# Who makes the low parts while the weights are split: a token mixer and two feed-forward networks in split fp32 on one core

## The chip, the cores and the metric

The kernel runs on one core of a Trainium2 chip. The metric is the device time of one execution in microseconds; a median of several executions is given. The profile is that of one further execution.

## What is computed

```python
w   = softmax over the 7 taps of weight            # 8 heads x 7 taps
x   = causal 7-tap mix of x along the sequence     # (2, 4096, 192), a head has 24 channels
g   = x @ w_gate;  v = x @ w_val                   # 8192 x 192 @ 192 x 1536
x   = (g * sigmoid(g) * v) @ w_out                 # 1536 x 192: the first network
h   = x @ w_in                                     # 192 x 2048
out = where(h > 0, h, exp(min(h, 0)) - 1) @ w_out2 # 2048 x 192: the second network
```

All in fp32. TensorE multiplies fp32r operands, so each fp32 operand is split into a high part, which is the value converted to fp32r, and a low part, the value less the high part. A product is then made of three: high x high, low x high and high x low.

## The kernel before

**Tiling.** The 8192 tokens go in 16 chunks of 512. For a chunk the seven taps are applied on VectorE (`mix`), the result is split into the input of the first network, which has 12 blocks of 128 hidden rows, and the output of that is split into the input of the second network, with 16 blocks worked in 8 pairs. The code calls the first network of chunk n `mix_phase(n)`, because the taps of chunk n + 1 are applied beside it, and its second `elu_phase(n + 1)`. The order is mix_phase(0), mix_phase(1), elu_phase(1) (the second network of chunk 0), mix_phase(2), and a loop over the rest. The stretch from about 90 to 129 us of the trace is elu_phase(1), chunk 0's second network.

**One block of the first network.** TensorE projects gate and value into two PSUM banks (`project`, 18 matmuls of 512 columns); ScalarE makes the silu of the gate (line 557); VectorE multiplies it with the value into `hidden` (line 734, 128x512, two buffers); ScalarE converts that into `hid_hi` (line 574, a ring of four); an engine subtracts the two into `hid_lo` (a ring of four; GpSimd, line 441); TensorE multiplies both with the output weights three blocks later (`down1`, 10 matmuls). The bank of block f is free for block f + 2 once its product is made.

**One pair of the second network.** TensorE projects two blocks. VectorE takes the minimum with 0 of both (line 771), ScalarE the exponential (line 593), VectorE the ELU of both (line 787), ScalarE the high parts (line 608), GpSimd the low parts (line 441). `down2_pair` multiplies a pair two pairs later (32 matmuls). A pair's projection waits for the ELUs of the pair two before.

**The weights** come in 18 pieces of at most 768 columns through six staging buffers. Of each piece ScalarE makes the high part (`make_hi`, line 319) and GpSimd the low part (`make_lo`, line 326); one piece, out2's third (index 16), is VectorE's. Five pieces are made ahead of block 0, and the others "beside" certain blocks: a table names the block after whose own work both engines do which piece.

```python
BESIDE0 = {1: 5, 3: 6, 5: 7, 7: 8, 8: 9}              # first network of chunk 0
BESIDE1 = {0: 10, 1: 11, 9: 12, 10: 13, 11: 14}       # first network of chunk 1
BESIDE_ELU1 = {3: 15, 4: 16, 5: 17}                   # pairs of the second network
```

TensorE waits for the first n pieces, high and low, ahead of the block that first reads them (`wait_weights`): in elu_phase(1) piece 15 ahead of pair 6's projection, piece 16 ahead of the down pair of blocks 8 and 9, piece 17 ahead of that of 12 and 13 in mix_phase(2).

**The order** on each engine is that of its code; engines wait for each other by counting semaphores. In chunk 0 VectorE does, per block, the product and two tap instructions of chunk 1 (blocks 2 to 8), and the halo copy at block 9. ScalarE makes the high halves of chunk 1's input after block 9's high part, when all of `mix` is done (`input1_hi`, line 515), VectorE then its low halves (`input1_lo`, line 696), and SyncE copies the first half of each crosswise (`cross1`, line 365). In elu_phase(1) ScalarE makes the same high halves for chunk 2 after the high parts of blocks 8 and 10, VectorE the low halves after the minimums of pairs 5 and 6. GpSimd sums halves of the first network's output between its low parts (`sum_y_tail`, `sum_y_main`, `fold_y_tail`, line 445). SyncE's queue issues in order the loads of weights and of x; the load of chunk 2's x waits until the transposes of chunk 1's (`transpose_x`, line 708) have read the buffer.

Of the kernel before, what the change touches and what calls it, by code (L numbers as in the profile page):

```python
# [22 lines left out]
F32 = mybir.dt.float32  # L23
# [8 lines left out]
def mix_ffn_ffn(nc, x, weight, w_gate, w_val, w_out1, w_in2, w_out2, out):  # L32
# [39 lines left out]
    with ctx:  # L72
# [119 lines left out]
        piece_lo_dve = sem("piece_lo_dve")  # L192
        piece_lo_pool = sem("piece_lo_pool")
# [51 lines left out]
        def up1_piece(g, who):  # L245
# [4 lines left out]
            pieces.append((loads, [(hi, s)], [(lo, s, hi)], who))  # L250

        def up2_piece(j0, j1, who):
# [4 lines left out]
            pieces.append((loads, [(hi, s)], [(lo, s, hi)], who))  # L257

        def out_piece(rows, dst, q, order, who):
# [4 lines left out]
            pieces.append((loads, [(t[:, :, 0:D], s)], los, who))  # L264

        def out1_piece(q):
            out_piece(wo1_rows, out1_w, q, [(D, P, TAIL), (D + TAIL, 0, P)], "pool")

        UP1_AT, OUT1_AT = {}, {}
        for what, at, who in (("up", 0, "pool"), ("up", 1, "pool"), ("up", 2, "pool"), ("out", 0, "pool"),  # L270
                              ("up", 3, "pool"), ("up", 4, "pool"), ("out", 1, "pool"), ("up", 5, "pool"),
                              ("up", 6, "pool"), ("out", 2, "pool")):
            if what == "up":
                up1_piece(at, who)
# [7 lines left out]
        for what, at, who in (("up", 0, "pool"), ("up", 2, "pool"), ("out", 0, "pool"), ("up", 4, "pool"),  # L282
                              ("out", 1, "pool"), ("up", 6, "pool"), ("out", 2, "dve"), ("out", 3, "pool")):
            if what == "up":
                up2_piece(at, at + 2, who)
                UP2_AT[at] = len(pieces)
            else:
                out_piece(wo2_rows, out2_w, at, [(D, 0, D)], who)
                OUT2_AT[at * OT] = len(pieces)

        AHEAD, READY = 6, 5
        BESIDE0 = {1: 5, 3: 6, 5: 7, 7: 8, 8: 9}
        BESIDE1 = {0: 10, 1: 11, 9: 12, 10: 13, 11: 14}
        BESIDE_ELU1 = {3: 15, 4: 16, 5: 17}
        assert READY + len(BESIDE0) == PIECES1
# [5 lines left out]
        def lo_count(upto, who):  # L301

            return sum(len(p[2]) for p in pieces[:upto] if p[3] == who)

        def wait_weights(eng, upto):

            eng.wait_ge(piece_hi, upto)
            for who, made in (("dve", piece_lo_dve), ("pool", piece_lo_pool)):
                if lo_count(upto, who):
                    eng.wait_ge(made, lo_count(upto, who))  # L310
# [10 lines left out]
        def make_lo(eng, i, who):  # L321
            if pieces[i][3] != who:
                return
            eng.wait_ge(piece_hi, i + 1)
            for dst, src, hi in pieces[i][2]:
                ins = eng.tensor_tensor(dst, src, hi.bitcast(F32), ALU.subtract)  # L326
                ins.then_inc(piece_lo_dve if who == "dve" else piece_lo_pool, 1)
# [91 lines left out]
        def _(pool):  # L419
# [44 lines left out]
            def mix_phase(n, extra=lambda f: None):  # L464
                for f in range(N1):
                    pool.wait_ge(hi1_done, N1 * n + f + 1)
                    lo_of(f % 2, f % RING).then_inc(lo1_done, 1)
                    if f == 2 and is_int(n, 1):
                        sum_y_tail(0)
                    if f == 3 and is_int(n, 1):  # L470
                        sum_y_main(0)
                    if f == 6 and is_int(n, 1):
                        fold_y_tail(0)
                    extra(f)

            def elu_phase(n, extra=lambda j: None):
                last = is_int(n, CHUNKS)
                for k in range(N2 - last):
                    pool.wait_ge(hi2_done, N2 * (n - 1) + k + 1)
                    lo_of(k % 2, k % RING).then_inc(lo2_done, 1)  # L480
                    if k == 3 and not last:
                        sum_y_tail(n)
                    if k == 5 and not last:
                        sum_y_main(n)
                    if k == 9 and not last:
                        fold_y_tail(n)
                    if k % 2:
                        extra(k // 2)

            for i in range(READY):  # L490
                make_lo(pool, i, "pool")
            lo = lambda i: make_lo(pool, i, "pool")
# [167 lines left out]
        def _(v):  # L660
# [60 lines left out]

            def mix_phase(n):
                lead = isinstance(n, int)
                for f in range(N1):
# [119 lines left out]
            elu_phase(1, beside(BESIDE_ELU1, lambda i: make_lo(v, i, "dve")))  # L844
# [258 lines left out]
```

## Time and profile before

| | us |
|---|---|
| median of 3 runs (lowest, highest) | 1205.79 (1205.67, 1207.7) |
| the profiled execution | 1206.76 |
| its span in the trace | 1205.0 |
| TensorE matmuls busy | 1199.5 (100%) |
| VectorE busy | 775.5 (64%) |
| ScalarE busy | 664.2 (55%) |
| GpSimd busy | 717.9 (60%) |

The span is the time from the first to the last instruction of the trace; the execution's own time has 1.76 us around it. The granted clock of TensorE is 1.0 of full speed throughout. Busy shares are averages over stages; a wait of TensorE shows as idle time in front of a row of its timeline, with the instruction that released it.

### The profile page before, as it was taken

The numbers are of one execution on the slowest core, as the hardware profiler recorded it, in microseconds if no ns is written. First come the engines' busy times: TensorE is split into PE (matmuls) and PEld (weight loads), VectorE is DVE, ScalarE is ACT, GpSimd is POOL, SyncE is SP. The second block draws the span as 40 slices with busy tenths as digits, with TensorE's granted clock in tenths as the row PEclk, the third lists the DMA queues.
The fourth block names the chain that finished last, engine by engine and source line by source line (L and its number), as shares of the span: only waits on it lengthen the run. The fifth ranks groups of instructions, "written<-read, shape, count | busy, mean of one in ns | idle before, by whom it ended". The sixth has DMA issues, their size and how long they took to land.

```text
span 1205.0 us, 31390 instructions
## 1 busy us (share of the span) xinstructions
PE 1199.5 (100%) x11798; PEld 1032.4 (86%) x11798; DVE 775.5 (64%) x1178; ACT 664.2 (55%) x1114; POOL 717.9 (60%) x528
## 2 busy tenths in 40 slices
PE   9999999999999999999999999999999999999999
PEld 7988888888888888889888898888988889888898
DVE  6787575675656756567665666656666476675665
ACT  6456555465554645546455464655546556465565
POOL 6787656574654746547465474654746557465565
PEclk9999999999999999999999999999999999999999
DMA  7412012120111211012110121100212002120110
GB/s 179 109 51 44 12 27 41 32 44 11 32 31 30 44 30 23 21 30 44 30 27 17 30 44 30 35 17 22 44 30 41 11 22 44 30 44 9 30 34 15
DMA packets 103955, 43.37 MB, mean 36 GB/s; under 512 B 75888, under 2 KB 93936, under 8 KB 103920
## 3 DMA queue, kind: packets, MB, share of 16 engines
q1 hardware_dynamic: 103104, 42.29, 15.7%
q10 hardware_dynamic: 816, 0.59, 0.2%
q8 instruction: 24, 0.39, 0.1%
q14 instruction: 11, 0.09, 0.0%
HBM read 16.12 MB, written 6.29 MB: 19 GB/s over the span
## 4 chain that ended last, share of the span: by engine, by line
PE 97%; POOL 1%; DVE 1%; issue 1%; ACT 0%; ACTq 0%; DVEq 0%
PE up L860 55%; PE down L860 42%; POOL hid_lo L441 1%; DVE mixed L830 0%; DVE act L771 0%; PE down L1063 0%; POOL up_w_lo L326 0%; DVE hidden L787 0%; ACT L617 0%; ACT hid_hi L608 0%; POOL y_main L445 0%; POOL halves L445 0%; DVE mixed L827 0%; DVE taps_head L813 0%; ACT act L593 0%
## 5 line engine op out<-in xcount | busy, mean ns | idle before, releaser
L441 POOL TENSOR_TENSOR hid_lo<-hidden,hid_hi 128x512 fp32r<-128x512 f32 x447 | 623.7, 1405 | 473.2 <-ACT hid_hi L574 304.8
L860 PE MATMUL down<-out_w,hid_hi 64*128 64x384 f32 x2040 | 300.4, 355 | 0.0
L734 DVE TENSOR_TENSOR hidden<-act,up 128x512 f32<-128x512 f32 x191 | 130.8, 685 | 249.1 <-ACT act L557 249.1
L860 PE MATMUL down<-out_w,hid_lo 64*128 64x192 f32 x2040 | 260.8, 251 | 0.3 <-POOL hid_lo L441 0.3
L771 DVE TENSOR_SCALAR act<-up 128x512 f32<-128x512 f32 x256 | 164.8, 685 | 112.0 <-PE up L860 112.0
L860 PE MATMUL up<-in_b_hi,up_w_hi 64*128 64x512 f32 x1128 | 224.1, 393 | 0.0
L860 PE MATMUL up<-in_b_hi,up_w_lo 64*128 64x512 f32 x1128 | 223.7, 393 | 0.0
L860 PE MATMUL up<-in_b_lo,up_w_hi 64*128 64x512 f32 x1128 | 223.6, 393 | 0.0
L574 ACT ACTIVATE hid_hi<-hidden 128x512 fp32r<-128x512 f32 x192 | 121.5, 633 | 177.9 <-DVE hidden L734 160.5
L608 ACT ACTIVATE hid_hi<-hidden 128x512 fp32r<-128x512 f32 x256 | 156.9, 628 | 96.5 <-DVE hidden L787 79.4
L593 ACT ACTIVATE act<-act 128x512 f32<-128x512 f32 x256 | 156.1, 631 | 94.8 <-DVE act L771 94.8
L860 PEld LDWEIGHTS down<-out_w,hid_lo 64*128 64x128 f32 x2040 | 196.1, 187 | 6.1 <-POOL hid_lo L441 0.6
L557 ACT ACTIVATE act<-up 128x512 f32<-128x512 f32 x191 | 114.0, 597 | 155.5 <-PE up L860 153.6
L860 PEld LDWEIGHTS down<-out_w,hid_hi 64*128 64x128 f32 x2040 | 192.6, 184 | 5.4 <-issue 0.3
L787 DVE SCALAR_TENSOR_TENSOR hidden<-act,up 128x512 f32<-128x512 f32 x256 | 168.8, 680 | 34.4 <-POOL hid_lo L441 25.4
L860 PE MATMUL down<-hid_hi,out_w 64*128 64x512 f32 x1152 | 165.4, 391 | 0.0
L860 PE MATMUL up<-in_a_hi,up_w_hi 64*128 64x512 f32 x786 | 159.7, 398 | 0.4 <-DVE hidden L787 0.4
L860 PE MATMUL up<-in_a_lo,up_w_hi 64*128 64x512 f32 x786 | 156.8, 391 | 0.0
L860 PE MATMUL up<-in_a_hi,up_w_lo 64*128 64x512 f32 x786 | 156.2, 389 | 0.0
L690 DVE SCALAR_TENSOR_TENSOR mixed<-x_t,taps,mixed 128x512 f32<-128x512 f32 x192 | 146.2, 802 | 0.0
L860 PEld LDWEIGHTS down<-hid_hi,out_w 64*128 64x128 f32 x1152 | 110.5, 186 | 24.7 <-issue 0.4
L860 PEld LDWEIGHTS up<-in_b_lo,up_w_hi 64*128 64x128 f32 x1128 | 106.8, 185 | 24.6
(96 smaller groups left out, 1085.9 us busy)
## 6 DMA issues: line engine op xcount, KB each, us to landing
x_raw<-x_dram SPq DMA_DIRECT2D x136, 64.0 KB, 2.2
out_dram<-stage SPq DMA_DIRECT2D x15, 384.0 KB, 2.7
in_b_hi<-in_b_hi SPq DMA_DIRECT2D x32, 128.0 KB, 2.3
in_b_lo<-in_b_lo SPq DMA_DIRECT2D x32, 128.0 KB, 2.3
swapped<-halves SPq DMA_DIRECT2D x32, 128.0 KB, 2.3
in_a_hi<-in_a_hi SPq DMA_DIRECT2D x30, 128.0 KB, 2.3
in_a_lo<-in_a_lo SPq DMA_DIRECT2D x30, 128.0 KB, 2.3
stage<-w_out_dram SPq DMA_DIRECT2D x7, 384.0 KB, 3.9
```

Source lines behind the costliest of these rows:

```text
L441: return pool.tensor_tensor(hid_lo[:, slot, :], hidden[:, s, :], hid_hi[:, slot, :].bitcast(F32), ALU.subtract)
L557: nc.scalar.activation(act[:, f % 2, :], gate_bank(f, n)[:, :], ACT.Silu)\
L574: nc.scalar.activation(hid_hi[:, f % RING, :], hidden[:, f % 2, :], ACT.Copy)\
L593: nc.scalar.activation(act[:, k % 2, :], act[:, k % 2, :], ACT.Exp).then_inc(exp_done, 1)
L608: nc.scalar.activation(hid_hi[:, k % RING, :], hidden[:, k % 2, :], ACT.Copy)\
L690: v.scalar_tensor_tensor(mixed[:, part, :], src, tap, mixed[:, part, :], ALU.mult, ALU.add).then_inc(mix_step, 1)
L734: v.tensor_tensor(hidden[:, f % 2, :], act[:, f % 2, :], val_bank(f, n)[:, :], ALU.mult)\
L771: v.tensor_scalar(act[:, k % 2, :], elu_bank(k)[:, :], 0.0, None, ALU.min)\
L787: v.scalar_tensor_tensor(hidden[:, k % 2, :], act[:, k % 2, :], -1.0, elu_bank(k)[:, :], ALU.add, ALU.max).then_inc(elu_done, 1)
L860: return nc.tensor.matmul(dst, lhsT, rhs, start=start, stop=stop, skip_group_check=True)
```

## The change

In chunk 0's first network the low parts of all 12 blocks are made by VectorE (`chunk0_lo`), each after the next block's product, the last after block 11; GpSimd leaves them out. The transposes of chunk 1's x go from block 1 to block 2, the two taps per block from blocks 2 to 8 to blocks 3 to 9; the halo copy stays at block 9. Piece 5 is made beside block 2 instead of block 1.

In elu_phase(1) the low parts of pairs 3, 4 and 5 (blocks 6 to 11) are made by VectorE, one pair later: after the minimums (and the input's low half) of pairs 4, 5 and 6 and before their ELUs. GpSimd leaves them out. Piece 16 goes from VectorE to GpSimd, and all low parts of weights are counted by one semaphore, `piece_lo`, instead of two.

```diff
-        BESIDE0 = {1: 5, 3: 6, 5: 7, 7: 8, 8: 9}
+        BESIDE0 = {2: 5, 3: 6, 5: 7, 7: 8, 8: 9}
...
+        DVE_LO1 = (3, 4, 5)
...
         def wait_weights(eng, upto):
             eng.wait_ge(piece_hi, upto)
-            for who, made in (("dve", piece_lo_dve), ("pool", piece_lo_pool)):
-                if lo_count(upto, who):
-                    eng.wait_ge(made, lo_count(upto, who))
+            eng.wait_ge(piece_lo, lo_count(upto))
...
 # GpSimd, mix_phase
-                    pool.wait_ge(hi1_done, N1 * n + f + 1)
-                    lo_of(f % 2, f % RING).then_inc(lo1_done, 1)
+                    if not is_int(n, 0):
+                        pool.wait_ge(hi1_done, N1 * n + f + 1)
+                        lo_of(f % 2, f % RING).then_inc(lo1_done, 1)
...
 # GpSimd, elu_phase
-                    pool.wait_ge(hi2_done, N2 * (n - 1) + k + 1)
-                    lo_of(k % 2, k % RING).then_inc(lo2_done, 1)
+                    if not (is_int(n, 1) and k // 2 in DVE_LO1):
+                        pool.wait_ge(hi2_done, N2 * (n - 1) + k + 1)
+                        lo_of(k % 2, k % RING).then_inc(lo2_done, 1)
...
 # VectorE, mix_phase
+            def chunk0_lo(f):
+                v.wait_ge(hi1_done, f + 1)
+                lo_of(f).then_inc(lo1_done, 1)
...
                     v.tensor_tensor(hidden[:, f % 2, :], act[:, f % 2, :], val_bank(f, n)[:, :], ALU.mult)\
                         .then_inc(mul_done, 1)
+                    if is_int(n, 0) and f >= 1:
+                        chunk0_lo(f - 1)
...
-                    if f == 1 and is_int(n, 0):
+                    if f == 2 and is_int(n, 0):
                         transpose_x(1, 0)
                         transpose_x(1, 1)
...
-                    at = 2 if is_int(n, 0) else 3
-                    if f == at - 1:
+                    if f == 2:
                         mix(n + 1, 0)
-                    if at <= f < at + TAPS:
-                        mix(n + 1, 2 * (f - at) + 1)
-                        mix(n + 1, 2 * (f - at) + 2)
-                    if f == at + TAPS:
+                    if 3 <= f < 3 + TAPS:
+                        mix(n + 1, 2 * (f - 3) + 1)
+                        mix(n + 1, 2 * (f - 3) + 2)
+                    if f == (9 if is_int(n, 0) else 10):
                         mix(n + 1, MIX - 1)
...
+                if is_int(n, 0):
+                    chunk0_lo(N1 - 1)
...
 # VectorE, elu_phase, after the minimums and input1_lo, before the ELUs
+                    for k in (2 * j - 2, 2 * j - 1):
+                        if is_int(n, 1) and k // 2 in DVE_LO1:
+                            v.wait_ge(hi2_done, k + 1)
+                            lo_of(k).then_inc(lo2_done, 1)
...
-            elu_phase(1, beside(BESIDE_ELU1, lambda i: make_lo(v, i, "dve")))
+            elu_phase(1)
```

## Rows read from the trace of the kernel before

**Rows 1.** The page, engines: busy us (share of the span) xinstructions.

```profile
PE 1199.5 (100%) x11798; PEld 1032.4 (86%) x11798; DVE 775.5 (64%) x1178; ACT 664.2 (55%) x1114; POOL 717.9 (60%) x528
```

**Rows 2.** Timeline of TensorE, chunk 0: start us, us, engine line operation [idle before <-releaser].

```profile
22.17 0.40 PE L860 MATMUL up<-in_a_lo,up_w_hi 64*128 64x512 f32 x2
22.59 0.96 PE L860 MATMUL down<-hid_hi,out_w 64*128 64x512 f32 x6
...
23.82 0.42 PE L860 MATMUL up<-in_a_hi,up_w_hi 64*128 64x512 f32 x2
...
27.07 0.44 PE L860 MATMUL up<-in_a_hi,up_w_hi 64*128 64x512 f32 x2
...
49.88 0.91 PE L860 MATMUL down<-hid_hi,out_w 64*128 64x512 f32 x6
...
51.05 0.45 PE L860 MATMUL up<-in_b_hi,up_w_hi 64*128 64x512 f32 x2
```

**Rows 3.** Timeline of TensorE, chunk 0's second network.

```profile
109.78 0.44 PE L860 MATMUL up<-in_a_hi,up_w_hi 64*128 64x512 f32 x2
...
114.17 0.44 PE L860 MATMUL up<-in_a_hi,up_w_hi 64*128 64x512 f32 x2
...
116.28 0.39 PE L860 MATMUL down<-out_w,hid_hi 64*128 64x384 f32 x2
...
119.19 0.50 PE L860 MATMUL up<-in_a_hi,up_w_hi 64*128 64x512 f32 x2 [0.40 <-DVE hidden L787]
...
122.32 0.36 PE L860 MATMUL down<-out_w,hid_lo 64*128 64x192 f32 x2 [0.31 <-POOL hid_lo L441]
...
124.23 0.42 PE L860 MATMUL up<-in_b_hi,up_w_hi 64*128 64x512 f32 x2
```

**Rows 4.** Timeline of VectorE, chunk 0's second network.

```profile
107.70 1.29 DVE L771 TENSOR_SCALAR act<-up 128x512 f32<-128x512 f32 x2 [0.94 <-PE up L860]
...
112.50 3.63 DVE L326 TENSOR_TENSOR out_w<-stage,out_w 128x768 fp32r<-128x768 f32 x1 [1.97 <-ACT out_w L319]
...
117.26 0.68 DVE L696 TENSOR_TENSOR in_b_lo<-mixed,in_b_hi 128x512 fp32r<-128x512 f32 x1
```

**Rows 5.** Timeline of VectorE, chunk 0.

```profile
39.77 1.40 DVE L690 SCALAR_TENSOR_TENSOR mixed<-x_t,taps,mixed 128x512 f32<-128x512 f32 x2
...
46.18 1.77 DVE L696 TENSOR_TENSOR in_b_lo<-mixed,in_b_hi 128x512 fp32r<-128x512 f32 x1 [0.70 <-ACT in_b_hi L515]
```

**Rows 6.** Timeline of GpSimd, chunk 0.

```profile
46.11 1.30 POOL L326 TENSOR_TENSOR out_w<-stage,out_w 128x512 fp32r<-128x512 f32 x1
47.37 1.74 POOL L441 TENSOR_TENSOR hid_lo<-hidden,hid_hi 128x512 fp32r<-128x512 f32 x1
```

**Rows 7.** Timeline of GpSimd, chunk 0's second network.

```profile
111.51 2.56 POOL L441 TENSOR_TENSOR hid_lo<-hidden,hid_hi 128x512 fp32r<-128x512 f32 x2
114.01 1.30 POOL L445 TENSOR_TENSOR y_tail<-halves,swapped 128x512 f32<-128x512 f32 x1
...
122.23 1.85 POOL L326 TENSOR_TENSOR out_w<-stage,out_w 128x768 fp32r<-128x768 f32 x1
```

**Rows 8.** Timeline of SyncE's queue of DMA issues, chunk 0.

```profile
20.96 5.16 SPq L345 DMA_DIRECT2D x_raw<-x_dram  x8
...
47.98 1.11 SPq L365 DMA_DIRECT2D in_b_lo<-in_b_lo  x2
```

**Rows 9.** The page, DMA issues: engine op xcount, KB each, us to landing.

```profile
in_b_lo<-in_b_lo SPq DMA_DIRECT2D x32, 128.0 KB, 2.3
```

**Rows 10.** Timeline of ScalarE, chunk 0.

```profile
21.03 0.58 ACT L557 ACTIVATE act<-down 128x512 f32<-128x512 f32 x1
```

**Rows 11.** Timeline of ScalarE, chunk 0's second network.

```profile
107.33 0.83 ACT L319 ACTIVATE up_w_hi<-stage 128x768 fp32r<-128x768 f32 x1
...
110.60 0.61 ACT L515 ACTIVATE in_b_hi<-mixed 128x512 fp32r<-128x512 f32 x1
...
111.64 0.83 ACT L319 ACTIVATE out_w<-stage 128x768 fp32r<-128x768 f32 x1
```

More of the change, by code:

```diff
@@ L191, in mix_ffn_ffn @@
         piece_hi = sem("piece_hi")
-        piece_lo_dve = sem("piece_lo_dve")
-        piece_lo_pool = sem("piece_lo_pool")
+        piece_lo = sem("piece_lo")
         gate_ready = sem("gate_ready")
@@ L243, in mix_ffn_ffn, with up1_piece @@
         pieces = []
-        def up1_piece(g, who):
+        def up1_piece(g):
             c0, c1 = GROUPS[g]
@@ L249, in up1_piece, with up2_piece @@
             hi, lo = up1_w["hi"][:, :, c0:c1], up1_w["lo"][:, :, c0:c1]
-            pieces.append((loads, [(hi, s)], [(lo, s, hi)], who))
-        def up2_piece(j0, j1, who):
+            pieces.append((loads, [(hi, s)], [(lo, s, hi)]))
+        def up2_piece(j0, j1):
             s = stage[:, len(pieces) % STAGES, 0:PARTS * (j1 - j0) * P].rearrange("p (g c) -> p g c", g=PARTS)
@@ L256, in up2_piece, with out_piece @@
             hi, lo = up2_w["hi"][:, :, j0 * P:j1 * P], up2_w["lo"][:, :, j0 * P:j1 * P]
-            pieces.append((loads, [(hi, s)], [(lo, s, hi)], who))
-        def out_piece(rows, dst, q, order, who):
+            pieces.append((loads, [(hi, s)], [(lo, s, hi)]))
+        def out_piece(rows, dst, q, order):
             s = stage[:, len(pieces) % STAGES, 0:OT * D].rearrange("p (f d) -> p f d", d=D)
@@ L263, in out_piece @@
             los = [(t[:, :, to:to + n], s[:, :, of:of + n], t[:, :, of:of + n]) for to, of, n in order]
-            pieces.append((loads, [(t[:, :, 0:D], s)], los, who))
+            pieces.append((loads, [(t[:, :, 0:D], s)], los))
         def out1_piece(q):
-            out_piece(wo1_rows, out1_w, q, [(D, P, TAIL), (D + TAIL, 0, P)], "pool")
+            out_piece(wo1_rows, out1_w, q, [(D, P, TAIL), (D + TAIL, 0, P)])
         UP1_AT, OUT1_AT = {}, {}
-        for what, at, who in (("up", 0, "pool"), ("up", 1, "pool"), ("up", 2, "pool"), ("out", 0, "pool"),
-                              ("up", 3, "pool"), ("up", 4, "pool"), ("out", 1, "pool"), ("up", 5, "pool"),
-                              ("up", 6, "pool"), ("out", 2, "pool")):
+        for what, at in (("up", 0), ("up", 1), ("up", 2), ("out", 0),
+                         ("up", 3), ("up", 4), ("out", 1), ("up", 5), ("up", 6), ("out", 2)):
             if what == "up":
-                up1_piece(at, who)
+                up1_piece(at)
                 UP1_AT[GROUPS[at][0] // P] = len(pieces)
@@ L281, in mix_ffn_ffn @@
         UP2_AT, OUT2_AT = {}, {}
-        for what, at, who in (("up", 0, "pool"), ("up", 2, "pool"), ("out", 0, "pool"), ("up", 4, "pool"),
-                              ("out", 1, "pool"), ("up", 6, "pool"), ("out", 2, "dve"), ("out", 3, "pool")):
+        for what, at in (("up", 0), ("up", 2), ("out", 0), ("up", 4),
+                         ("out", 1), ("up", 6), ("out", 2), ("out", 3)):
             if what == "up":
-                up2_piece(at, at + 2, who)
+                up2_piece(at, at + 2)
                 UP2_AT[at] = len(pieces)
             else:
-                out_piece(wo2_rows, out2_w, at, [(D, 0, D)], who)
+                out_piece(wo2_rows, out2_w, at, [(D, 0, D)])
                 OUT2_AT[at * OT] = len(pieces)
         AHEAD, READY = 6, 5
-        BESIDE0 = {1: 5, 3: 6, 5: 7, 7: 8, 8: 9}
+        BESIDE0 = {2: 5, 3: 6, 5: 7, 7: 8, 8: 9}
         BESIDE1 = {0: 10, 1: 11, 9: 12, 10: 13, 11: 14}
         BESIDE_ELU1 = {3: 15, 4: 16, 5: 17}
+        DVE_LO1 = (3, 4, 5)
         assert READY + len(BESIDE0) == PIECES1
@@ L299, in beside, with lo_count @@
             return lambda at: make(table[at]) if at in table else None
-        def lo_count(upto, who):
-            return sum(len(p[2]) for p in pieces[:upto] if p[3] == who)
+        def lo_count(upto):
+            return sum(len(p[2]) for p in pieces[:upto])
         def wait_weights(eng, upto):
             eng.wait_ge(piece_hi, upto)
-            for who, made in (("dve", piece_lo_dve), ("pool", piece_lo_pool)):
-                if lo_count(upto, who):
-                    eng.wait_ge(made, lo_count(upto, who))
+            eng.wait_ge(piece_lo, lo_count(upto))
         def stage_full(i):
@@ L319, in make_hi, with make_lo @@
                 nc.scalar.activation(dst, src, ACT.Copy).then_inc(piece_hi, 1)
[L321 to L324, printed above, removed]
+        def make_lo(pool, i):
+            pool.wait_ge(piece_hi, i + 1)
             for dst, src, hi in pieces[i][2]:
-                ins = eng.tensor_tensor(dst, src, hi.bitcast(F32), ALU.subtract)
-                ins.then_inc(piece_lo_dve if who == "dve" else piece_lo_pool, 1)
+                pool.tensor_tensor(dst, src, hi.bitcast(F32), ALU.subtract).then_inc(piece_lo, 1)
         def store_tokens(eng, m, blocks=slice(0, BLOCKS)):
@@ L490, in _ @@
             for i in range(READY):
-                make_lo(pool, i, "pool")
-            lo = lambda i: make_lo(pool, i, "pool")
+                make_lo(pool, i)
+            lo = lambda i: make_lo(pool, i)
             mix_phase(0, beside(BESIDE0, lo))
@@ L720, in add_z, with lo_of @@
                     v.tensor_tensor(result[:, b, :], result[:, b, :], Z[b][:, 0:D], ALU.add)                        .then_inc(result_done, 1)
+            def lo_of(f):
+                return v.tensor_tensor(hid_lo[:, f % RING, :], hidden[:, f % 2, :],
+                                       hid_hi[:, f % RING, :].bitcast(F32), ALU.subtract)
+            def chunk0_lo(f):
+                v.wait_ge(hi1_done, f + 1)
+                lo_of(f).then_inc(lo1_done, 1)
             def mix_phase(n):
```

## The prediction

> **What bounds the kernel now.** I read the page's engine shares first, then TensorE's timeline through the two stretches that the diff touches, then the timelines of the engines that feed it there, and last the rows where VectorE and GpSimd use SBUF at once. TensorE is busy for all but 5.5 us of the span [rows 1]. From chunk 2's first network on nothing in the diff differs, so only time that TensorE loses before about 125 us can change.
>
> In chunk 0 a block takes 3.25 us (27.07 less 23.82) [rows 2]. The matmuls from 22.17 would hand over at 22.40, and the down projection starts at 22.59: 0.19 us lost, waiting for the third multiplication. From 23.82 on eight periods and one more down projection (49.88 to 51.05, 1.17 us) give 50.99, and chunk 1's first projection starts at 51.05. So nothing more is lost in chunk 0.
>
> In chunk 0's second network a pair of blocks takes 4.39 us (109.78 to 114.17). The next two pairs take 5.02 (to 119.19) and 5.04 (to 124.23): 0.63 + 0.65 = 1.28 us lost [rows 3]. The first loss is VectorE's own piece of weights, out2's third: 3.63 us at 112.50 [rows 4], in front of the minimums of pair 5. The second is GpSimd's low part of block 11, which came late for the same reason. **So the most that the change can give is 1.28 + 0.19 = 1.47 us, 0.12%.** A measurement of this kernel can tell about 0.2%, 2.4 us, from no change.
>
> **Part 1: chunk 0's twelve low parts go to VectorE.** Price of one: alone, the same instruction on VectorE takes 0.68 us (at 117.26 [rows 4]). Beside GpSimd it took 1.77: it started at 46.18, GpSimd's instruction of 46.11 ended at 47.41, and it ended 0.54 later, at 47.95 [rows 5, 6]; GpSimd's next, issued at 47.37, took 1.74 where 1.30 is its time alone. So whoever comes second waits, and the two take turns. These are the two ends; I take 0.68 where the walk finds GpSimd idle and "end of GpSimd's instruction + 0.54" where not.
>
> GpSimd keeps only five pieces in chunk 0: 1.85, 2.03, 1.85, 1.0 and 2.03, 8.8 us (a piece of 768 columns is 1.85 [rows 7]; a 512 part is 1.30 [rows 6], the rest by its columns). VectorE's work in blocks 3 to 9 is 7 x (0.69 + 0.68) for product and low part and 14 taps at 0.70 (1.40 for two [rows 5]), 19.4 us, in seven periods of 3.25, 22.8. Walking it with a product no earlier than 2.9 us after its projection begins (2.1 of matmuls, 0.2 to the silu, 0.6 of silu), and with GpSimd's piece starting after ScalarE's high part and piece: the waits behind GpSimd are 1.2 us (block 3), 1.2 (block 4), 1.2 (block 6), 0.9 (block 7) and 0.75 (block 9). The product of block 9 runs at 42.8 to 43.4, low part 8 ends at 44.7, the two last taps at 46.1, the halo copy at 46.3. That is 1.2 us later than in the kernel before, whose taps were one block ahead. ScalarE's high halves follow at 46.9 and 47.5, and the two low halves at 47.6 and 48.3, now with GpSimd idle (before: 1.77 each). TensorE reads them at 50.85. The crossed halves are tightest: the high pair is issued at 46.9, the low pair at about 48.1 instead of 47.98 [rows 8], 1.11 us of issue and 2.3 to land [rows 9]: 51.5, and TensorE reaches that slot 1.39 after 50.85, at 52.24. **Part 1 costs nothing, with 0.7 us of cover at the crossed halves**; without it each us late costs one.
>
> The low parts for TensorE have more: low 9 ends at 49.6, needed at 50.4; low 10 and 11 at 52.3 and 52.9, needed at 53.6 and 54.8. The products are 2 us or more ahead of the projection that reuses their bank.
>
> **Part 2: piece 5 and the transposes move from block 1 to block 2.** ScalarE's silu of block 2 no longer waits behind a piece; it began at 21.03 [rows 10] and can begin at 20.4. The product of block 2 then ends near 21.7, not 22.3, and the 0.19 us go: **gain 0.2**. Bounds: 0 and 0.2. The load of chunk 2's x, which waited for the transposes (issued from 20.96 [rows 8]), starts some 2.7 us later, and with it the twelve w_in loads behind it on SP's queue. They are first read at 55 us; nothing waits. Piece 5 is read by block 7, at 33.6, and is ready at 25. On GpSimd's queue, low part 0 and 1 no longer stand in front of it.
>
> **Part 3: pairs 3, 4, 5 of chunk 0's second network.** VectorE gives up its 3.63 us and takes six low parts; GpSimd gives up six and takes the piece. The walk, on the clock of the trace before:
> - Pair 4. Minimums 107.70 to 108.99 [rows 4]. GpSimd, free of low 6 and 7, does up2's last piece as soon as ScalarE has its high part (107.33 + 0.83 = 108.16 [rows 11]): 108.2 to 110.0. Low 6 waits for it: ends 110.6. GpSimd's next, the sum of y's tail (1.30 [rows 7], at 114.01 before), now comes at 110.0, waits for low 6 and ends at 111.7; low 7 ends at 112.3. ELU 8 and 9 end at 112.9 and 113.5.
> - ScalarE behind them (0.6 for a high part, as at 110.60): high 8, 112.95 to 113.55; chunk 2's high half (0.61 [rows 11]) to 114.1; high 9 to 114.65; then out2's third piece, 0.83, to 115.4. Before it began at 111.64.
> - Pair 5. VectorE: minimums 113.5 to 114.75, input's low half to 115.4, low 8 to 116.0. GpSimd's piece 16 waits for low 8 and runs 115.95 to 117.8. TensorE needs that piece at 116.28 [rows 3]: **it waits 1.55 us**. Low 9, behind the piece, ends at 118.35, ELU 10 and 11 at 119.0 and 119.6. TensorE ends the down pair and starts pair 7 at 120.15 (before: 119.19).
> - Pair 6. ScalarE: high 10, input's high half, high 11, piece 17: to 121.5. VectorE: minimums 119.5 to 120.8, input's low half to 121.4, low 10 to 122.05. GpSimd's last piece waits for it and ends at 123.85, low 11 at 124.4. TensorE wants low 11 at 122.26 + 0.47 = 122.73: **1.7 us more**. Its next projection, chunk 2's first, starts at 126.3; before at 124.23.
>
> From there GpSimd makes the low parts again, and ELU 14 and 15 (to 128.95) are ahead of TensorE's 130.7. So part 3 gives back the 1.28 and loses 3.3: +2.05 us. The two stalls of before go; a queue on VectorE takes their place, about 4.66 us of work alone per pair of 4.39 (four passes 2.56, two low parts 1.36, one half of the input 0.68, transfers of turn aside).
>
> **Sum:** 0 - 0.2 + 2.05 = +1.85 us. The profiled execution is 1206.76 (span 1205.0, 1.76 around it), so 1208.6 on its own base. It is 0.97 above the median of three, 1205.79; I forecast the median: 1205.79 + 1.85 = 1207.6, within 0.2%.
>
> **A rule against the trace.** The row at 112.50 shows VectorE's piece of 768 columns taking 3.63 us while GpSimd's three instructions from 111.51 to 115.31 each kept their time alone [rows 4, 7]: VectorE waited through all three. The Trainium skill (SBUF — State Buffer, Who interferes with whom) has an exclusive lock: the second to issue fully blocks until the first finishes. By that the piece had been done near 113.7, and the trace agrees at 46.18 but not at 112.50. It also advises to schedule in such a case whichever is off the critical path, which speaks against low parts on VectorE beside GpSimd's pieces. In my walk turns (46.18) give low 7 at 112.3; waiting out back-to-back instructions (112.50) gives low 6 at 111.9 and low 7 at 112.5, +0.25 us. I take turns, which the shape at 46.18 shows, and keep both.
>
> **Rivals.**
> - Light contention (chance 0.27). If low 6 and 7 pass GpSimd without waiting, they end at 110.3, high 9 at 112.75, piece 16 at 115.4, before TensorE's 116.28; low 11 ends at 119.8, before 120.7. All of the 1.28 and 0.2 is gained: 1205.79 - 1.5 = 1204.3. For it: two low parts at 0.68 fit between the minimums and the ELUs, and the two taps from 39.77 took 1.40 untouched [rows 5], though GpSimd was at work in that chunk. Against: GpSimd's piece starts at 108.2, before low 6 at 108.95. Half a case, only the second stall missed, is 1205 to 1206.
> - Chunk 1's input late (0.17), the slower side. VectorE's 19.4 us and GpSimd's 8.8 in blocks 3 to 9 are 28.2 us if they never overlap, against 22.8. That is at most 5.4 late, less the 0.7 of cover, 4.7. It decides from the point where the last tap ends after 46.8; TensorE's first projection of chunk 1 then waits for the crossed halves. Its likely size, half of it, 2.3 us, on top of +1.85: 1209.9. Against: the products and silus leave gaps in which GpSimd runs alone.
> - The queue on VectorE costs a good deal less, because a piece and a low part fall in the other order (0.10): +0.5, 1206.3.
>
> **How the numbers follow.** Forecast 0.46, light contention 0.27, late input 0.17, other order 0.10. Low end: the full gain, 1204.3. High end: +1.85 with half of what the late input can cost, 1210.0. Slower by over 0.2% means above 1208.2: the late input, and about a quarter of the forecast, whose two waits can be 0.6 longer: 0.17 + 0.10 = 0.27. Faster by over 0.2% has no mechanism here (1.47 is the most); 0.03 is for what the runs themselves spread (1205.67 to 1207.7). The rest, 0.70, is within 0.2%.
>
> **What would show it.** Right: no gap at 22.4; VectorE's taps in chunk 0 ending near 46; in the second network TensorE waiting before the down pair of blocks 8 and 9 for GpSimd's out_w, over 1 us, and within the pair of 10 and 11 for VectorE's hid_lo; the piece's high part on ScalarE after 114. Wrong: neither wait there and pairs of 4.39 throughout (light contention), or a wait of TensorE near 51 to 52 us for the crossed halves.

## The result and the profile after

The changed kernel takes 1209.54 us (median of 11, 1208.37 to 1209.99) against 1205.80 (median of 11, 1204.33 to 1207.7): ratio 1.0028, interval [1.0018, 1.0037]. That is **slower by 3.7 us between the medians, 0.28% by the ratio**, inside the stated range and outside the 0.2% that was the likeliest case.

The page has TensorE as busy as before [rows 1], VectorE 6 us busier and GpSimd 24 us less; the span is 1206.5 against 1205.0.

```profile
PE 1199.6 (99%) x11798; PEld 1032.2 (86%) x11798; DVE 781.3 (65%) x1195; ACT 664.4 (55%) x1114; POOL 694.0 (58%) x511
```

TensorE's timeline from chunk 0 to chunk 2's first projection (start us, us, engine line operation [idle before <-releaser]); the rows answer to [rows 2, 3]:

```profile
22.39 0.86 PE L871 MATMUL down<-hid_hi,out_w 64*128 64x512 f32 x6
...
50.75 0.41 PE L871 MATMUL up<-in_b_hi,up_w_hi 64*128 64x512 f32 x2
...
109.46 0.42 PE L871 MATMUL up<-in_a_hi,up_w_hi 64*128 64x512 f32 x1
...
114.00 0.42 PE L871 MATMUL up<-in_a_hi,up_w_hi 64*128 64x512 f32 x2
...
117.40 0.45 PE L871 MATMUL down<-out_w,hid_hi 64*128 64x384 f32 x2 [1.13 <-issue]
...
119.83 0.42 PE L871 MATMUL up<-in_a_hi,up_w_hi 64*128 64x512 f32 x2
...
123.74 0.36 PE L871 MATMUL down<-out_w,hid_lo 64*128 64x192 f32 x2 [1.17 <-DVE hid_lo L719]
...
125.67 0.42 PE L871 MATMUL up<-in_b_hi,up_w_hi 64*128 64x512 f32 x2
```

The gap at 22.4 is gone and chunk 1 begins at 50.75, 0.30 earlier than before. The two old waits, 0.63 and 0.65, are gone too. In their place TensorE stops ahead of the down pair of blocks 8 and 9 (117.40; its weight loads had been idle 1.53 us; the profile names no releaser, and GpSimd's piece 16 ends at 117.30) and inside the pair of 10 and 11, for VectorE's `hid_lo` (123.74). Pairs that take 4.39 undisturbed take 5.83 (114.00 to 119.83) and 5.84 (to 125.67), and the one before them 4.54. Chunk 2 begins at 125.67 instead of 124.23: **+1.44 us**, and to the end both traces run in step.

The engines that feed it, VectorE, then GpSimd, then ScalarE, in the same columns; they answer to [rows 4, 7, 11]:

```profile
108.59 3.44 DVE L719 TENSOR_TENSOR hid_lo<-hidden,hid_hi 128x512 fp32r<-128x512 f32 x2
...
114.95 2.90 DVE L719 TENSOR_TENSOR hid_lo<-hidden,hid_hi 128x512 fp32r<-128x512 f32 x2
...
120.77 2.92 DVE L719 TENSOR_TENSOR hid_lo<-hidden,hid_hi 128x512 fp32r<-128x512 f32 x2
```

```profile
107.92 1.85 POOL L321 TENSOR_TENSOR up_w_lo<-stage,up_w_hi 128x768 fp32r<-128x768 f32 x1 [1.01 <-ACT up_w_hi L316]
109.73 1.74 POOL L439 TENSOR_TENSOR y_tail<-halves,swapped 128x512 f32<-128x512 f32 x1
115.14 2.16 POOL L321 TENSOR_TENSOR out_w<-stage,out_w 128x768 fp32r<-128x768 f32 x1 [3.67 <-ACT out_w L316]
120.97 2.17 POOL L321 TENSOR_TENSOR out_w<-stage,out_w 128x768 fp32r<-128x768 f32 x1 [3.67 <-ACT out_w L316]
```

```profile
112.66 0.63 ACT L604 ACTIVATE hid_hi<-hidden 128x512 fp32r<-128x512 f32 x1 [3.32 <-DVE hidden L798]
113.20 0.61 ACT L511 ACTIVATE in_b_hi<-mixed 128x512 fp32r<-128x512 f32 x1
...
114.24 0.83 ACT L316 ACTIVATE out_w<-stage 128x768 fp32r<-128x768 f32 x1
```

Each pair of low parts costs VectorE 3.44, 2.90 and 2.92 us where two alone are 1.28. In each case one of GpSimd's instructions is under way when the second low part of the pair is due (in the first case when the first is due, too): piece 15 and the sum of y's tail (107.92, 109.73), piece 16 (115.14), piece 17 (120.97). ScalarE can make the high part of piece 16 only at 114.24, against 111.64 [rows 11], since high 8 waited 3.32 us for its ELU.

### The profile page after: what moved, and what is told of

Same layout as the page of the kernel before. It is cut to its first block, busy times and chain, and to the rows that moved or that the text cites. A ratio compares the mean times of both kernels' runs of the same rounds, so it can differ in the third digit from the quotient of the medians.

```text
span 1206.5 us, 31388 instructions
## 1 busy us (share of the span) xinstructions
PE 1199.6 (99%) x11798; PEld 1032.2 (86%) x11798; DVE 781.3 (65%) x1195; ACT 664.4 (55%) x1114; POOL 694.0 (58%) x511
## 4 chain that ended last, share of the span: by engine, by line
PE 98%; DVE 1%; issue 1%; ACT 0%; ACTq 0%; DVEq 0%
PE up L871 55%; PE down L871 43%; DVE hid_lo L719 0%; DVE act L778 0%; ACT L613 0%; DVE in_b_lo L692 0%; PE down L1074 0%; DVE taps_head L824 0%; ACT hidden L620 0%; DVE hidden L798 0%; ACTq L611 0%; ACT act L625 0%; DVE stage L716 0%; ACT stage L650 0%; ACT taps_exp L613 0%
## 5 line engine op out<-in xcount | busy, mean ns | idle before, releaser
L435 POOL TENSOR_TENSOR hid_lo<-hidden,hid_hi 128x512 fp32r<-128x512 f32 x429 | 597.2, 1402 | 473.9 <-ACT hid_hi L570 307.6
L686 DVE SCALAR_TENSOR_TENSOR mixed<-x_t,taps,mixed 128x512 f32<-128x512 f32 x192 | 141.1, 775 | 0.0
```

The lines of the kernel that those rows point to most:

```text
L435: return pool.tensor_tensor(hid_lo[:, slot, :], hidden[:, s, :], hid_hi[:, slot, :].bitcast(F32), ALU.subtract)
L686: v.scalar_tensor_tensor(mixed[:, part, :], src, tap, mixed[:, part, :], ALU.mult, ALU.add).then_inc(mix_step, 1)
```

## The experiments

The queue theory: VectorE's queue in chunk 0's second network, lengthened by waits behind GpSimd's pieces, is what costs. Its rivals: the work moved in chunk 0 costs; six more low parts are too much for VectorE whatever GpSimd does; part of the time is not in the engines' waits at all. The traces below start their first projection at 13.92 or 13.93, as before and after do, but for one, of which it is said. So the start of chunk 2's first projection (before 124.23, after 125.67) compares them.

**Chunk 0's part alone (e1).** The kernel before with every edit to chunk 0, and `BESIDE_ELU1`, the second network and piece 16 left as they were.

> The kernel before with the edits in chunk 0 alone: its twelve low parts on VectorE, transposes and piece 5 one block later, taps from block 3; the second network as before. Queue theory (the loss comes from VectorE's queue in chunk 0's second network): span 1204.7, that is 1205.0 less the 0.3 us that chunk 0 gained in the changed kernel, and the two old waits of TensorE, 0.63 and 0.65, still there. Rival (moving the work in chunk 0 costs): some of the 1.5 us of added span shows here, above 1205.2. Time around the span: if it is the number of semaphores, as before (1.8 us, so 1206.5 in time); if it is the added code in chunk 0, 3 us as in the changed kernel.

1206.73, ratio 1.0003 [0.9994, 1.0012]; span of the trace 1204.7.

```profile
22.39 0.86 PE L872 MATMUL down<-hid_hi,out_w 64*128 64x512 f32 x6
...
50.74 0.40 PE L872 MATMUL up<-in_b_hi,up_w_hi 64*128 64x512 f32 x2
...
118.83 0.50 PE L872 MATMUL up<-in_a_hi,up_w_hi 64*128 64x512 f32 x2 [0.40 <-DVE hidden L799]
...
123.89 0.42 PE L872 MATMUL up<-in_b_hi,up_w_hi 64*128 64x512 f32 x2
```

Chunk 2 begins 0.34 earlier than before, both old waits still there. As expected; the time around the span is 1.8 us. The median is all the same 0.6 us above that of the kernel before: its spans have a median of 1205.0 against 1204.1, of which more below.

**The second network's part alone (e2).**

```diff
+        DVE_LO1 = (3, 4, 5)
...
-                              ... ("out", 2, "dve"), ...
+                              ... ("out", 2, "pool"), ...
...
```

The rest of the edit is that of the changed kernel's second network: VectorE makes the low parts of these pairs and GpSimd leaves them out.

> The kernel before with the edits in chunk 0's second network alone: low parts of blocks 6 to 11 on VectorE, piece 16 on GpSimd. Queue theory: the two old waits go, a wait of about 1.4 us ahead of the down pair of blocks 8 and 9 and one of about 1.4 us inside the pair of 10 and 11 come; span 1205.0 + 1.76 = 1206.8, the slowest of this group. Rival (moving the work in chunk 0 costs): 1205.0 to 1205.5. Time around the span: 1.8 us if it goes with the number of semaphores, 3 us if it goes with this part's code.

1209.34, ratio 1.0027 [1.0016, 1.0037]; span 1206.8.

```profile
22.59 0.96 PE L867 MATMUL down<-hid_hi,out_w 64*128 64x512 f32 x6
...
51.06 0.45 PE L867 MATMUL up<-in_b_hi,up_w_hi 64*128 64x512 f32 x2
...
114.33 0.42 PE L867 MATMUL up<-in_a_hi,up_w_hi 64*128 64x512 f32 x2
...
117.73 0.44 PE L867 MATMUL down<-out_w,hid_hi 64*128 64x384 f32 x2 [1.12 <-issue]
...
120.16 0.42 PE L867 MATMUL up<-in_a_hi,up_w_hi 64*128 64x512 f32 x2
...
125.99 0.42 PE L867 MATMUL up<-in_b_hi,up_w_hi 64*128 64x512 f32 x2
```

+1.76 at chunk 2, and -0.34 + 1.76 = 1.42 is the changed kernel's 1.44: the two parts add, and the trace's loss is all in the second network. The time around the span was not as expected: 1.7 or 1.8 us in three of eight executions, 2.3 to 2.9 in five.

**The kernel before again (n1)**, as a measure of the comparison itself (no edit).

> The kernel before once more, run in the place of a changed one. It tells what part of the 3.7 us is the comparison's own. If the three spans that the kernel before shows (1202.6, 1203.7 to 1204.3, 1205.1 to 1205.6) and the 1.8 to 2.2 us around them belong to the kernel, its median is 1206.1 again and the ratio 1.000. If they belong to the place in the order of runs, its spans are 1205.0 or more in most runs and its median 1207.

1206.48, ratio 0.9998 [0.9989, 1.0007], its spans from 1202.4 to 1205.3 like those of the 33 beside it. The place in the order does nothing that can be seen.

**One more semaphore (e4)** in the changed kernel, `unused = sem("unused")`.

> The changed kernel with one more semaphore declared that nothing uses, so that their number is that of the kernel before. Span 1206.5 as in the changed kernel. If the number of semaphores sets the time around the span, it is 1.8 to 2.2 us and the time 1208.3 to 1208.7; if not, 3.0 us and 1209.5.

1209.21, ratio 1.0026 [1.0016, 1.0035]; spans 1206.6 in the median as after, 2.9 us around them. The number of semaphores is not the cause; the run also repeats the changed kernel's time. What it shows beside that is a wait which the changed kernel's own trace does not have, of TensorE's weight loads for the crossed half of chunk 1's input:

```profile
52.27 0.19 PEld L872 LDWEIGHTS up<-in_b_hi,up_w_hi 64*128 64x128 f32 x2 [0.41 <-DMA in_b_lo<-in_b_lo]
```

**VectorE's low parts kept, pieces 15 and 16 early (e5).** The changed kernel, with two pieces three pairs earlier:

```diff
-        BESIDE_ELU1 = {3: 15, 4: 16, 5: 17}
+        BESIDE_ELU1 = {0: 15, 1: 16, 5: 17}
```

> The changed kernel, VectorE's six low parts kept, but pieces 15 and 16 beside pairs 0 and 1 of the second network; piece 17 stays beside pair 5. Queue theory, in which the waits behind GpSimd's pieces make VectorE late: no wait of TensorE ahead of the down pair of blocks 8 and 9, and the wait inside the pair of 10 and 11 stays, 1.0 to 1.7 us, for low part 11 stands behind piece 17 as before; span 1205.0 or so, 1.4 to 1.6 below the changed kernel. Rival (VectorE's six low parts by themselves are too much, 4.66 us of work in a pair of 4.39): TensorE waits at both places, span 1206.0 or more.

1205.78, ratio 0.9995 [0.9986, 1.0004]; span 1203.9. Chunk 2 begins at 122.75, 2.92 earlier than in the changed kernel, and **neither** wait is left, where one was expected to stay. VectorE, then GpSimd:

```profile
109.51 1.74 DVE L719 TENSOR_TENSOR hid_lo<-hidden,hid_hi 128x512 fp32r<-128x512 f32 x2
...
114.17 1.28 DVE L719 TENSOR_TENSOR hid_lo<-hidden,hid_hi 128x512 fp32r<-128x512 f32 x2
...
117.77 0.68 DVE L692 TENSOR_TENSOR in_b_lo<-mixed,in_b_hi 128x512 fp32r<-128x512 f32 x1
118.37 1.28 DVE L719 TENSOR_TENSOR hid_lo<-hidden,hid_hi 128x512 fp32r<-128x512 f32 x2
```

```profile
118.58 2.79 POOL L321 TENSOR_TENSOR out_w<-stage,out_w 128x768 fp32r<-128x768 f32 x1 [8.47 <-ACT out_w L316]
```

The low parts of pairs 4 and 5 take 1.28 for two. Piece 17 is issued at 118.58 while VectorE's run of three instructions with two SBUF inputs (117.77 to 119.65) is under way; this time GpSimd waits, 2.79 instead of 1.85, until the run is over. So the six low parts fit on VectorE once they are not late. Their seven instructions of a pair take 4.20 us when nothing holds them up (the minimums of 112.37 to those of 116.57), under the 4.39 of a pair: instructions that follow each other begin 0.60 apart, where the rival had counted their full durations. The rival of too much work falls.

```profile
112.37 1.27 DVE L778 TENSOR_SCALAR act<-up 128x512 f32<-128x512 f32 x2
...
116.57 1.28 DVE L778 TENSOR_SCALAR act<-up 128x512 f32<-128x512 f32 x2
```

That no second wait is left has two reasons. Low part 10 begins 0.01 us after pair 7's projection (118.36), and 0.94 after it in the changed kernel; and low part 11 did not wait out the piece. TensorE wants low part 11 2.48 after that projection. With a turn, as in the changed kernel, it would have ended 2.93 after it. So, by an estimate from these rows, lateness made about 0.9 of the second wait of 1.43, and about 0.5 was left to which of the two instructions got through.

**Piece 15 alone early (e8)**: `{0: 15, 4: 16, 5: 17}`.

> The changed kernel with one entry of the table moved: piece 15 beside pair 0 instead of pair 3, pieces 16 and 17 where they were. Theory of the chain (low parts 6 and 7 wait behind piece 15 and the sum of y's tail, that makes ELUs 8 and 9 late, then the high part of piece 16, then its low part): low parts 6 and 7 take 0.69 each, the piece's high part ends by 113.2 instead of 115.07, its low part by 115.6, against TensorE's need at 115.97; the first wait is gone or under 0.3 us, and the second, which the first lateness fed, is under 0.5; span 1203.6 to 1204.1. Rival (piece 16 and low parts 8 and 9 hold each other up by themselves): the first wait stays over 1 us and the second too, span 1206 or more.

1207.46, ratio 1.0012 [1.0003, 1.0021]; span 1205.2. VectorE, then the weight loads' waits:

```profile
108.62 1.28 DVE L719 TENSOR_TENSOR hid_lo<-hidden,hid_hi 128x512 fp32r<-128x512 f32 x2
...
113.61 2.94 DVE L719 TENSOR_TENSOR hid_lo<-hidden,hid_hi 128x512 fp32r<-128x512 f32 x2
...
119.46 2.92 DVE L719 TENSOR_TENSOR hid_lo<-hidden,hid_hi 128x512 fp32r<-128x512 f32 x2
```

```profile
116.60 0.19 PEld L871 LDWEIGHTS down<-out_w,hid_lo 64*128 64x128 f32 x2 [0.24 <-DVE hid_lo L719]
...
122.43 0.19 PEld L871 LDWEIGHTS down<-out_w,hid_lo 64*128 64x128 f32 x2 [1.43 <-DVE hid_lo L719]
```

The chain's first half is as expected: low 6 and 7 take 1.28 for two, piece 16's high part starts at 112.11, the wait ahead of the down pair of blocks 8 and 9 is gone and 0.24 remains inside it. Its second half is not: low 8 and 9 beside piece 16 take 2.94, low 10 and 11 beside piece 17 take 2.92, and the second wait is 1.43, as in the changed kernel; so the first wait is not what fed it. A piece that gets in between a pair of low parts costs VectorE about 1.6 us; piece 17 in e5, issued as far behind low part 10 (0.21 us, here 0.20), did not get in and cost it nothing. Why one did and the other not, no run shows. Three such meetings in three pairs made VectorE late in the changed kernel, and one taken away leaves one of the two waits.

**All low parts of the second network on GpSimd (e6)**: `DVE_LO1 = ()`, table unchanged.

> The changed kernel with all sixteen low parts of the second network on GpSimd again, the table of pieces unchanged, so GpSimd has piece 16 as well as the low parts. Queue theory: VectorE's queue is gone, but piece 16 stands behind low parts 8 and 9 and the sum of y's tail, 115.0 to 116.8, against TensorE's need at 115.97: one wait of 0.9 us, span 1204.3. Rival (GpSimd overfull, waits as long as in the changed kernel): 1206.0 or more.

1206.78, ratio 1.0002 [0.9993, 1.0011]; span 1206.0, where 1204.3 was expected. One wait as expected, 1.59 us ahead of the same down pair:

```profile
117.72 0.22 PEld L871 LDWEIGHTS down<-out_w,hid_hi 64*128 64x128 f32 x2 [1.59 <-issue]
```

```profile
114.12 1.75 POOL L439 TENSOR_TENSOR y_tail<-halves,swapped 128x512 f32<-128x512 f32 x1
115.83 1.83 POOL L321 TENSOR_TENSOR out_w<-stage,out_w 128x768 fp32r<-128x768 f32 x1
```

It is larger than the 0.9 expected, in part because the sum of y's tail takes 1.75 behind one of VectorE's instructions. This trace also waits 0.46 at 52, and after its last matmul, 0.3 later than before, it takes 0.7 longer than the kernel before to write its output: SyncE's last pair of issues takes 1.69 where it took 1.01. The pair with the wait takes 5.81 (114.29 to 120.10), so the new home of piece 16 alone costs 1.42, a little more than the old waits. The first wait of the changed kernel thus needs no queue on VectorE: GpSimd's own queue makes it as well.

**Pieces 15 and 16 early, all low parts of the second network on GpSimd**: with chunk 0's low parts on VectorE (e3), and with chunk 0 as before (e7).

> The changed kernel with all sixteen low parts of the second network on GpSimd again and pieces 15 and 16 beside its pairs 0 and 1, where GpSimd was idle, instead of 3 and 4. Queue theory: nothing on VectorE but its own passes, piece 16 ready ten microseconds early, no wait of TensorE from 24 us to the end of that network: span 1205.0 - 0.3 - 1.28 = 1203.4. Rival (GpSimd has no room for both low parts and pieces there): low parts of blocks 4 to 7 late by 1.9 us, a wait of TensorE of 1 us or more near 107 to 112, span 1204.4 or more.

> The kernel before, chunk 0 untouched, with piece 16 given to GpSimd and pieces 15 and 16 beside pairs 0 and 1. If the gain of the version with early pieces is that table's alone: span 1205.0 - 1.28 = 1203.7 from the same start, TensorE without a wait in the second network, and 0.3 above the version that has chunk 0's low parts on VectorE too. Rival (chunk 0's part is needed to make room): a wait remains, span 1204.4 or more.

1205.28, ratio 0.9994 [0.9985, 1.0003] (span 1202.3), and 1205.62, ratio 0.9993 [0.9984, 1.0002] (span 1203.8). Neither has a wait of TensorE in the second network. The second trace begins chunk 2 at 122.95, 1.28 earlier than before, as expected. The first starts 1.16 us earlier than all others (12.76) and begins it at 121.45, which is 122.61 from the common start, 0.34 ahead of the other. Both medians are some 4 us below the changed kernel's; against the kernel before they are 0.06% and 0.07% ahead, and the intervals reach just past 1, so a gain over it is seen in the traces alone.

What the three pairs from pair 5's projection to chunk 2's first one take, in the traces, with neither the start nor the wait at 52 in it:

| | low parts 6 to 11 | pieces 15, 16 beside pairs | us | over 13.17 |
|---|---|---|---|---|
| before | GpSimd | 3, 4 (16 on VectorE) | 14.45 | 1.28 |
| changed | VectorE | 3, 4 | 16.21 | 3.04 |
| e2 | VectorE | 3, 4 | 16.19 | 3.02 |
| e6 | GpSimd | 3, 4 | 14.58 | 1.41 |
| e8 | VectorE | 0, 4 | 14.86 | 1.69 |
| e5 | VectorE | 0, 1 | 13.17 | 0.00 |
| e7 | GpSimd | 0, 1 | 13.16 | 0.00 |

With the pieces early it makes no difference who has the low parts; with the pieces late, low parts on VectorE add 1.6 us to a loss that is there without them.

**Low part 8 behind the taps (e9)** in block 9 of chunk 0, on top of e3.

```diff
-                    if is_int(n, 0) and f >= 1:
+                    if is_int(n, 0) and f >= 1 and f != 9:
...
                     if f == 9 and is_int(n, 0):
+                        chunk0_lo(8)
                         input1_lo(1, 0)
```

> The version with all low parts of the second network on GpSimd and pieces 15 and 16 early, and in block 9 of chunk 0 VectorE makes low part 8 after the taps and the halo copy, in the gap where it waits for ScalarE's high half, instead of ahead of the taps. Theory (the crossed halves of chunk 1's input have next to no cover, since SyncE needs 1.4 to 1.8 us to issue the high pair): ScalarE's high half starts at 46.2 or earlier, SyncE issues the low pair by 48.7 and no execution waits for it; span 1203.4 from the late start, 1202.2 from the early one. Rival (the wait of 0.3 to 0.5 us on the crossed half has to do with the transfers' landing, not with when they are issued): it can appear here too.

1205.44, ratio 0.9993 [0.9984, 1.0002]; span 1203.9, 0.5 over what was expected. The theory fell. The high halves were ready 0.6 us earlier, and SyncE's queue lost it again. Its issues, TensorE's weight loads, and the packets between 47 and 48 us (queue, kind, packets, MB, share):

```profile
46.95 2.50 SPq L359 DMA_DIRECT2D in_b_hi<-in_b_hi  x2
49.51 1.22 SPq L359 DMA_DIRECT2D in_b_lo<-in_b_lo  x2
```

```profile
52.46 0.19 PEld L872 LDWEIGHTS up<-in_b_hi,up_w_hi 64*128 64x128 f32 x2 [0.45 <-DMA in_b_lo<-in_b_lo]
```

```profile
DMA packets 1, 0.02 MB, mean 16 GB/s; under 512 B 0, under 2 KB 0, under 8 KB 0
...
q8 instruction: 1, 0.02, 8.7%
```

The issue of the high pair takes 2.50 us, where it takes 1.17 from 46.17 in the kernel before, 1.39 from 47.58 in the changed kernel, and 1.68 and 1.84 from 47.6 in e4 and e6. So it ends at 49.45, no earlier than in the traces that begin it 0.6 us later (48.97 to 49.45). In the microsecond shown nothing moves but one transfer of instructions, at 47.7.

Such a transfer, and not the pause of SyncE ahead of the pair, is what the slow pairs have in common. In the thirteen traces of this document SyncE issues some 1000 pairs after the first 30 us, and 21 of them take more than 1.25 us. At each of the 21 a transfer of instructions begins between 0.3 us before the pair and 0.8 after its start, and the pair ends 1.3 to 1.9 us behind the transfer. A pause of over 5 us stands ahead of some 48 pairs in every trace, 25.7 us long in the loop, and all but at most two of these take 1.2 or less. Three pairs took 1.10 or 1.11 with a transfer that began 0.7 us or later in them, and four took 1.00 to 1.12 with one 0.2 to 0.3 ahead. That the queue waits for its own instructions fits these rows; no run was made that moves the transfer.

**The transposes back at block 1 (e10)**, on the version with pieces 15 and 16 early.

> The version with all low parts of the second network on GpSimd and pieces 15 and 16 early, with the transposes of chunk 1's x back at block 1 of chunk 0 (after low part 0). Theory (the crossed halves of chunk 1's input are late because the moved transposes held back the load of chunk 2's x and all that SyncE issues behind it): SyncE issues that load from 21 to 22, not 23.7, the high pair's issue near 47.6 takes 1.2 us as in the kernel before, and TensorE does not wait at 52. Rival (the slow issue has another cause, such as the pause of SyncE ahead of it): the pair takes 1.4 us or more again and a wait of 0.2 to 0.5 us can appear. Span 1203.4 from the late start in either case, plus 0.2 if the wait is there.

1205.63, ratio 0.9993 [0.9984, 1.0003]; span 1203.9. The load of x is issued at 21.66, and the high pair still takes 2.22 us, from 46.84. The moved transposes are not the cause. This trace has no wait at 52, which is between the two expectations.

## Why the prediction was right, and where it was wrong

**Part 3, the mechanism: right.** The walk named both places, their order and their cause, and e1 and e2 show that the trace's loss lies there and nowhere else. Its sizes on the clock of the trace before against those of the second part alone: high part of piece 16 at 114.65 (114.57); first wait 1.55 (1.53); pair 7 at 120.15 (120.16); second wait 1.7 (1.43); chunk 2 at 126.3 (125.99). The term was +2.05 and is +1.76. Low 11 did wait out all of piece 17, as walked, but ended at 124.02 and not 124.4: the walk gave VectorE's instructions some 0.65 us each, and back to back they begin 0.60 apart. The 4.66 us of work in a pair of 4.39, with which the prediction closes this part, is wrong for the same reason (its own terms add up to 4.60): e5 shows 4.20. In these traces VectorE's own work never filled a pair; with the waiting behind GpSimd it did.

**Part 2: right, under-sized**: 0.2 forecast, 0.30 at the start of chunk 1. The load of chunk 2's x was issued at 23.66, 2.7 us later as forecast, and TensorE waited for none of the weight loads behind it.

**Part 1: "costs nothing" holds in the trace of the changed kernel, but the 0.7 us of cover is not there.** Of the eight traces with chunk 0's low parts on VectorE and the transposes moved, five show TensorE waiting 0.21 to 0.46 for the crossed half; of the four with chunk 0 as before none does. The step that failed is "the low pair at about 48.1": it was issued at 49.02 in the changed kernel, because the high pair, issued at 47.58 and not 46.9, took 1.39. It was issued late because the taps ended at 46.8 and not 46.1, and they did because low part 8 ended at 45.48 and not 44.7. A price on the way there was misread: the walk gave every two taps 1.40, from the row at 39.77. GpSimd was idle when both began, from 38.70 to 40.59. Where it was at work in the same trace, two taps took 2.25 to 3.44, as in the first two rows here (GpSimd's, then VectorE's); the third is the changed kernel's, with GpSimd's piece at 38.99.

```profile
34.69 2.31 POOL L326 TENSOR_TENSOR up_w_lo<-stage,up_w_hi 128x768 fp32r<-128x768 f32 x1
35.80 3.44 DVE L690 SCALAR_TENSOR_TENSOR mixed<-x_t,taps,mixed 128x512 f32<-128x512 f32 x2
```

```profile
38.35 2.20 DVE L686 SCALAR_TENSOR_TENSOR mixed<-x_t,taps,mixed 128x512 f32<-128x512 f32 x2
```

How much of the lateness this price makes, and how much the longer wait of low part 8 itself (1.81 beside GpSimd's piece), was not told apart. The rival of a late input is real, but cost at most 0.46 of the 4.7 us that were counted as possible.

**Sum and base: the step that failed.** The forecast put the median at 1205.79 plus the change of the trace. The trace's change was +1.44 (forecast +1.85), the median's +3.7. So more than half of the measured loss is in no term of the sum. That 1209.5 still lies in the range is luck: the range ended at 1210.0 for the sake of the late input, which did not come. The spans and the times give the rest:

- Start. The kernel before has spans in three groups, in 96 executions beside the experiments: 1202.5 to 1203.1, 1203.2 to 1204.5, and 1205.0 to 1205.6; 31 of 96 in the last. The profiled execution that I read was of the last. The changed kernel's 11 are all but one at 1206.4 to 1207.1, its own last group. Medians: 1206.6 against 1204.0, 2.6 us, of which 1.44 is the waits. Counted in the same way, the last group holds most executions of every version with an edit (8 of 11 in e1, all 8 of e2, 9 of 11 in e3), 6 of 11 in e7 and 5 of 11 in the kernel run again. What sets one group apart from the next, two traces show: TensorE's timeline at the start, in the kernel before and then in e3.

```profile
5.30 1.97 PE L1063 MATMUL down<-ident,stage 128*128 128x128 f32 x8
...
13.93 0.50 PE L860 MATMUL up<-in_a_hi,up_w_hi 64*128 64x512 f32 x2
```

```profile
5.01 1.09 PE L1074 MATMUL down<-ident,stage 128*128 128x128 f32 x8
...
12.76 0.50 PE L871 MATMUL up<-in_a_hi,up_w_hi 64*128 64x512 f32 x2
```

The same eight transposes take 1.97 or 1.09 us, they begin 0.29 apart, and together this is the 1.17 us between the first projections. That the other executions' groups come from this too is argued from their distance; only these traces show it.

- Around the span: 2.0 us in the median before, 3.1 in the changed kernel (2.9 in its twin with one more semaphore).

So of 3.7 us some 1.4 is TensorE waiting for other engines, some 1.2 the group of the span and some 1.0 the time around it (differences of medians, so they need not add exactly). That the last two belong to the kernel and not to the comparison is shown by the kernel run again (0.9998) and by the twin (1.0026). Their cause is open. More than 2.8 us around the span are found only where VectorE makes low parts in the second network: in 8 of 11 executions of the changed kernel, 6 of 10 of the twin, 1 of 8 in e2, 3 of 11 in e5 and 3 of 10 in e8. The other versions reach 2.79 and the kernel before 2.39. It was not tried what in the program does it.

**The rivals.** Light contention fell in the changed kernel, and e5 shows what it would have been: 1.28 for two, no wait. The taps at 39.77, which spoke for it, were no sign, since GpSimd was idle when both of them began.

**Who waits for whom.** The Trainium skill (SBUF — State Buffer, Who interferes with whom) has a VectorE instruction with two inputs in SBUF and a GpSimd instruction that reads SBUF exclude each other: the one that issues second waits for the first. The runs agree where two instructions meet: GpSimd's piece at 115.14 in the changed kernel waits for low part 8, issued 0.19 before it, and low part 9 for the piece. For how long, the runs show more than one instruction: VectorE waited through three of GpSimd's [rows 4, 7], and GpSimd's piece 17 in e5 through low parts 10 and 11, though the second was issued after it. Turns were taken at 109.7, 115.1 and 121.0 in the changed kernel. The Trainium skill also advises, on the same page (Summary: rules for kernel authors), to schedule whichever of the two is off the critical path. The early pieces do that with GpSimd's part, and 1209.5 us became 1205.8 (e5).

## What to carry to other kernels

Work taken off a busy engine comes back if what is left there collides with it: a weight split of 1.85 us cost VectorE some 1.6 us when it got in between a pair of low parts, and moving two splits three pairs earlier, into idle time of the same engine, gave in the trace all the 1.28 us that moving the low parts was to give (e7). Take the price of an instruction from a row in which the other engine is known to be at work, or known to be idle, and say which. Ask of each queue that gets work what stands behind it in chains through the other engines: here VectorE's delay of 3 us reached ScalarE, and through it GpSimd's piece. When the expected change is 0.1%, one trace is not the base: look at the spans of many executions first.

## What was not expected of the hardware

- Back-to-back instructions of one engine can keep the other out to the end of their run, in either direction: 3.63 us for VectorE [rows 4], 2.79 instead of 1.85 for GpSimd (e5).
- A pair of DMA issues on SyncE's queue takes 1.10 to 1.15 us in most places, even after a pause of 25.7 us. It took 1.3 to 2.5 us in 21 places of thirteen traces, each with a transfer of instructions beside its start; nine of them are the high pair of chunk 1's input, and five of these made TensorE wait. Whether the queue waits for its own instructions is not shown.
- The same eight transposes at the start take 1.97 or 1.09 us with the granted clock at 1.0 in both.
